# A gated two-layer kernel on one core: 66 instead of 128 weight columns for the low part of g, and another warm-up series

## The reference, cut to what matters

```python
def _attn_ref(x, weight):              # x (4, 4096, 192), weight (8, 7)
    w = softmax(weight)                # over the 7 taps of each head
    x_pad = zeros(6 rows) + x          # along the sequence
    out[b, s, h, g] = sum_k w[h, k] * x_pad[b, s + k, h, g]

def _moe_ref(x, w_in, w_out):          # (16384, 192), (192, 2048), (2048, 192)
    h = x @ w_in
    g = h * np.cos(h)
    return (g @ w_out).astype(np.float32)

def _moe2_ref(x, w_in, w_out):
    h = x @ w_in
    relu6 = np.clip(h + 3.0, 0.0, 6.0)
    g = h * relu6 / 6.0
    return (g @ w_out).astype(np.float32)

def reference(...):
    return _moe2_ref(_moe_ref(_attn_ref(x, weight)))
```

## Time and profile before

| what | value |
|---|---|
| median of 3 runs | 2409.83 us (2409.76 to 2409.97) |
| the profiled execution's own time | 2408.54 us |
| its span | 2406.8 us |
| mean granted clock of TensorE | 0.995 of full |
| busy: TensorE, weight loads | 2367.1 us, 1929.2 us |
| busy: VectorE, ScalarE, GpSimd | 1776.7 us, 1495.7 us, 1313.7 us |
| products, each with its weight load | 10,254 |

### The profile page before, as it was taken

The page is one execution under the profiler, slowest core; times in us unless marked ns, Lnnn a source line. Parts: engine busy times, 40 slices in busy tenths (PEclk is TensorE's granted clock), DMA queues, the critical chain, the costliest instruction groups (busy, mean ns, idle before and its releaser), DMA issues.

```text
span 2406.8 us, 32826 instructions
## 1 busy us (share of the span) xinstructions
PE 2367.1 (98%) x10254; PEld 1929.2 (80%) x10254; DVE 1776.7 (74%) x2253; ACT 1495.7 (62%) x1748; POOL 1313.7 (55%) x543
## 2 busy tenths in 40 slices
PE   5999999999999999999999999999999999999998
PEld 3788888888888888888888888888888888888886
DVE  8777776777767777767777677777677776777753
ACT  4765566665666655666656666566666566665663
POOL 6755555555555555555555555555555555555554
PEclk8999999999999999999999999999999999999999
DMA  4100000000000000000000000000000000000001
GB/s 110 38 1 13 7 7 13 13 13 13 0 13 13 13 13 7 7 13 13 13 13 0 13 13 13 13 6 7 13 13 13 13 0 13 13 13 13 3 4 20
DMA packets 208226, 32.76 MB, mean 14 GB/s; under 512 B 203088, under 2 KB 207184, under 8 KB 208208
## 3 DMA queue, kind: packets, MB, share of 16 engines
q1 hardware_dynamic: 208208, 32.53, 7.7%
HBM read 19.92 MB, written 12.58 MB: 14 GB/s over the span
## 4 chain that ended last, share of the span: by engine, by line
PE 97%; DVE 1%; issue 1%; DMA 1%; SPq 0%; ACT 0%; POOL 0%; DVEq 0%; POOLq 0%; ACTq 0%
PE h_ps L347 10%; PE h_ps L346 10%; PE acc L366 10%; PE acc_tail L368 10%; PE h_ps L349 10%; PE acc L365 10%; PE acc_tail L369 10%; PE h_ps L348 10%; PE h_ps L350 10%; PE acc L367 10%; DMA gate<-in_moe_w_out 1%; DVE pre L520 0%; DVE gate L533 0%; DVE in_ftail L580 0%; DVE in_f L580 0%
## 5 line engine op out<-in xcount | busy, mean ns | idle before, releaser
L690 POOL TENSOR_TENSOR g_lo<-gate,g_hi 128x1024 fp32r<-128x1024 f32 x512 | 1270.2, 2481 | 1070.0 <-ACT g_hi L442 1069.7
L428 ACT ACTIVATE pre<-h_ps,three 128x1024 f32<-128x1024 f32 x256 | 286.7, 1120 | 547.0 <-PE h_ps L350 547.0
L442 ACT ACTIVATE g_hi<-gate 128x1024 fp32r<-128x1024 f32 x512 | 538.8, 1052 | 31.7 <-DVE gate L533 31.2
L520 DVE TENSOR_TENSOR pre<-pre,h_ps 128x1024 f32<-128x1024 int32 x256 | 311.9, 1218 | 257.3 <-ACT pre L426 257.3
L535 DVE SCALAR_TENSOR_TENSOR gate<-pre,h_ps 128x512 f32<-128x512 f32 x512 | 327.3, 678 | 214.5 <-ACT pre L428 213.5
L533 DVE TENSOR_TENSOR gate<-pre,h_ps 128x512 f32<-128x512 f32 x512 | 331.6, 685 | 129.4 <-ACT pre L436 126.0
L346 PE MATMUL h_ps<-in_hi,win_hi 128*128 128x512 f32 x1024 | 406.1, 397 | 18.7 <-DVE gate L533 9.9
L426 ACT ACTIVATE pre<-h_ps 128x1024 int32<-128x1024 f32 x256 | 262.4, 1025 | 232.5 <-PE h_ps L350 232.5
L347 PE MATMUL h_ps<-in_lo,win_hi 128*128 128x512 f32 x1024 | 406.1, 397 | 0.0
L349 PE MATMUL h_ps<-in_tail,wtail_hi 128*128 128x512 f32 x1024 | 403.4, 394 | 0.0
L366 PE MATMUL acc<-g_lo,wout 128*128 128x512 f32 x1024 | 402.6, 393 | 0.0
(11 more groups left out here) (69 smaller groups left out, 2225.8 us busy)
## 6 DMA issues: line engine op xcount, KB each, us to landing
x_in<-in_x SPq DMA_DIRECT2D x128, 64.0 KB, 2.2
out_dram<-o_blk SPq DMA_DIRECT2D x128, 64.0 KB, 1.8
blk_tail<-in_x SPq DMA_DIRECT2D x64, 64.0 KB, 2.2
out_dram<-blk_tail SPq DMA_DIRECT2D x64, 64.0 KB, 1.8
stage<-in_moe_w_out SPq DMA_DIRECT2D x6, 384.0 KB, 3.2
stage<-in_moe_w_in SPq DMA_DIRECT2D x3, 512.0 KB, 3.7
stage<-in_moe_w_in SPq DMA_DIRECT2D x6, 256.0 KB, 4.1
gate<-in_moe_w_out SPq DMA_DIRECT2D x2, 384.0 KB, 12.2
```

The lines of the kernel that those rows point to most:

```text
L442: act.activation(g_hi[:, q % G_BUFS, :], gate[:, q % 2, :], ACT.Copy).then_inc(ghi_ready, 1)
L690: pool.tensor_tensor(g_lo[:, n, :], gate[:, q % 2, :], g_hi[:, n, :].bitcast(F32), ALU.subtract).then_inc(glo_ready, 1)
```

## The change

Two things are changed.

1. In `second_product` the low part of g is multiplied with the 64 columns of the tail's high part and 2 more columns (`NARROW = 66`) instead of all 128. The product of the low part of g with 62 of the 64 columns of the tail's low part is no longer computed. In the last half of a phase the narrow product comes ahead of the wide one, so that the wide one ends the sum on all 128 partitions.
2. `warm_up` waits for the first rounded weights as before, and for the taps' copies (`taps_ready`) instead of nine convolution steps. It issues 62 products instead of ten: whole ones (128 rows, 128 columns), pairs of two that use rows 0 to 63 and rows 64 to 127 into two banks, four with 66 columns and four with 64.

```diff
-WARM_PRODUCTS = 10
-WARM_STEP = 9
+NARROW = 66
...
-                    pe.matmul(acc_tail[pair][:, :], w[:, P:2 * P], hi, start=first, stop=False)
-                    last = pe.matmul(acc_tail[pair][:, :], w[:, P:2 * P], lo, start=False, stop=final)
+                    if not final:
+                        pe.matmul(acc_tail[pair][:, :], w[:, P:2 * P], hi, start=first, stop=False)
+                    last = pe.matmul(acc_tail[pair][0:NARROW, :], w[:, P:P + NARROW], lo, start=False, stop=False)
+                    if final:
+                        last = pe.matmul(acc_tail[pair][:, :], w[:, P:2 * P], hi, start=False, stop=True)
                 last.then_inc(mix_done, 1)
...
                 pe.wait_ge(whi_done, 1)
-                pe.wait_ge(conv_step, WARM_STEP)
-                for _ in range(WARM_PRODUCTS):
-                    pe.matmul(h_ps[:, 1, TOK:W], win_hi[L1][:, 0:P], win_hi[L1][:, 0:TOK], start=True, stop=True)
+                pe.wait_ge(taps_ready, 2)
+                top, low, all_rows = slice(0, DT), slice(DT, P), slice(0, P)
+
+                def product(rows, cols, bank):
+                    pe.matmul(h_ps[0:cols, bank, TOK:W], win_hi[L1][rows, 0:cols], win_hi[L1][rows, 0:TOK],
+                              start=True, stop=True)
+
+                for _ in range(12):
+                    product(all_rows, P, 1)
+                for _ in range(4):
+                    product(top, P, 0)
+                    product(low, P, 1)
+                    for _ in range(3):
+                        product(all_rows, P, 1)
+                for _ in range(6):
+                    product(top, P, 0)
+                    product(low, P, 1)
+                for _ in range(4):
+                    product(all_rows, P, 1)
+                for _ in range(4):
+                    product(all_rows, NARROW, 1)
+                for _ in range(3):
+                    product(all_rows, P, 1)
+                for _ in range(4):
+                    product(all_rows, DT, 1)
+                for _ in range(3):
+                    product(all_rows, P, 1)
```

## The result

The change made the kernel slower: a median of 2423.48 us (2421.99 to 2424.07, six runs) against 2409.90 us (six runs of the kernel before on the same chip). The ratio is 1.0055, 95% interval 1.0042 to 1.0068, so 13.6 us were added. The forecast was no change, 2409.8, within 2392.5 to 2414.0. It was wrong in kind, and the time lies outside the range.

What follows compares the result with a forecast made beforehand. The tensor engine's time from product to product, 230.0 ns, was taken as the bound. Narrow product, order and warm-up summed as 0 + 0 + 0 = 0, giving 2409.8 us, range 2392.5 to 2414.

Steps and rivals of the forecast that it cites:

- The reading of the 17 ns: TensorE's long run: 17 of 230 ns per product are not stream and go with load and product, whatever the width.
- The first rival: In L369 the weight load gates the product, so a narrow load saves 17 ns each: 2393 us, chance 28%.
- its second value: The load-gates-product case by the Trainium skill's page: 14.2 ns saved per narrow product, 14 us in all, 2395 us.
- the second (2401.6): Rival for L369: the 17 ns excess is a share of the load's columns, saving 8 us: 2401.6 us, chance 10%.
- part 1: 66 instead of 128 weight columns in L369, 1024 times: cost 0, bounds 17 us gain and 112 or 223 us loss.
- a broken overlap at 112 us: L369's narrow form not overlapping its neighbours: 0.11 us of a restart once per narrow product, 112 us in all.
- the warm-up's 2414: Upper end of the range, from the new warm-up's bound of +3 us at the start of the kernel.
- The slower rival: At L369 the narrow form breaks the overlap with neighbours, on one side (2522) or both (2633), chance 10%.
- the 0.34 us of a restart: Time from first product to successor when TensorE restarts at 37.03 us, instead of 0.23; expected around L369 if overlap broke.
- Its test: Broken overlap is decided if the gap before or behind L369 grows at all; 5 ns would show.
- Parts 2 and 3: Narrow product before wide in a phase's last half, cost 0; new warm-up, cost 0, bounds -1 and +3 us.
- the expected signs for the start: First real product between 27.04 and 30 us, and VectorE's first subtraction of a fraction still at 34.2 us.

Runs made afterwards that it cites:

- all operands in step: Kernel before with 192 unused bytes ahead of in_f, putting inputs and weights at the same place modulo 256 bytes: 2376.46 us; with the 66-column product too, 2376.58 us.
- distance 64: Inputs left where the kernel before has them, 64 bytes from the weights' place modulo 256 bytes: 2409.95 us for the kernel before.

## Why the prediction was wrong

**The reading of the 17 ns was right.** The load does not gate the product. A load recorded for 0.14 instead of 0.19 gave nothing, neither in the change nor with all operands in step. The first rival (2393, or 2395 by its second value) and the second (2401.6) both fall with this.

**The step that failed is part 1's "cost 0" and its bounds.** I took the excess over the stream's 213 ns as something that goes with a pair of load and product "whatever its width", thus as a constant. It is not: of the 17 ns, 13.3 stay when all operands are in step (226.6 to 226.7), and the other 3.3 are a mean over products that depends on where their operands lie and on the products before them. The narrow slice changed this second part, by 26.7 ns per slot of 20, or 13.3 ns for each narrow product. My bounds had no row for that: 17 ns of gain, and on the other side a broken overlap at 112 us. Between 0 and 112 us I had nothing, so the range ended at the warm-up's 2414.

**The slower rival had the sign and not the mechanism.** No overlap broke: the load of L369 begins with the product before it as ever, and L369 never stood the 0.34 us of a restart from its neighbours. Its test was the useful part of it: any growth "before or behind L369" decides, since nothing covers it. The growth was behind, in the five products that follow the first narrow one of a slot, 1.13 to 1.16; these 25 ns are nearly all of the slot's 26.7.

**The rows could have warned me.** The kernel before had groups of five at 1.13 and at 1.16 in every slot. I checked that the mean was 230.0 over 10,090 products, and took a mean for a pace. A group that is faster than its twins, with the same shapes, says that something else than shape has a part in the time.

**Parts 2 and 3 were right.** The order cost nothing (ratio 1.0000), and so did the warm-up (1.0000). Its series ended at 28.7, inside 26.2 to 34.1. The weight loads of its last part show what the changes of form cost:

```profile
22.62 1.24 PEld L408 LDWEIGHTS h_ps<-win_hi 64*128 64x128 f32 x12 [0.37 <-issue]
24.22 4.01 PEld L408 LDWEIGHTS h_ps<-win_hi 128*128 128x128 f32 x18 [0.36 <-issue]
```

Between the pairs of 64 rows and the whole products around them the loads stood still for 0.37 and 0.36 us, where 0.04 is usual (0.24 to 0.37 at all such changes at full clock). The 18 loads behind that are of 128, 66, 128, 64 and 128 columns, and take 4.01 us, thus 0.23 from one to the next: the changes of width cost nothing. The twelve of 64 rows are six pairs, and a pair passes in some 0.23, as one whole product does. The first real product came at 30.29 rather than by 30, and VectorE's subtraction at 35.99 rather than 34.2, because VectorE's steps were slow; the expected signs for the start were bound to one execution, and it varies by 2 us.

**What stays open.** Distance 0 modulo 256 bytes as the fast place of the inputs is shown by four distances and two places of the same distance. But the pads moved the inputs alone, with all weights at 128 past a multiple of 256. The weights' place counts too: with the moving operand where it was, a full slice shifted by 62 or 32 columns cost 9 and 6 us. Whether it is the distance between the two that counts, or that each begins at 128 past a multiple of 256, no run tells; moving inputs, g and weights together would. What in the memory's read path makes it so was not tried. Nor do I have a rule for partial slices: from the same first column, 127 columns cost 3.3 us, 96 cost 4.7 and 66 cost 13.3, while 66 in one half cost 1.7 or nothing. In the kernels moved by 64 and by 192 bytes the 66 columns were free. In the first of these the first products were out of step as well, so neighbours out of step are not enough to make a narrow slice cost; why it costs with the inputs at distance 64 and not at 128 stays open. Widths other than 66 were tried at distance 64 alone.

## What to carry to other kernels

Where TensorE is the bound, compare groups of equal products with each other before you trust a mean: a pace that differs at equal shape can be time to be had. Look at the addresses of the moving operand and of the weights; here a pad of 192 bytes, putting both at the same place modulo 256 bytes, was worth 1.4%. And making a weight slice narrower gave nothing here beside a stream of 512 columns, at any of three distances, and at one of them it cost 13.3 us.

## What the runs showed of the hardware

- A product of 512 columns in fp32r with its own load of 128 weight columns took between 226.6 ns (both operands at distance 0) and 231.3 ns as a mean over the kernel, at full clock throughout, with only addresses and one slice of the weights changed.
- Slots of 20 products repeated to the nanosecond: 4599 to 4600 ns before, 4626 to 4627 after, in each of some 500 slots of both layers, so that neither the work of the other engines nor the layer shows in it.
- The effect has memory. The five second products right behind the first products took 1.16 us where the next five took 1.13, at the same addresses modulo 256 bytes. With the inputs at distance 0 all twenty took 1.13 per five.
- The pace at half clock showed none of this: 426 ns, the stream alone.
- A load of 66 columns is recorded for 0.14 us against 0.19 for 128, and brought nothing: 9,796 products in 2220 us with either.
- In the warm-up's series, changes between 128, 66 and 64 weight columns left the loads 0.23 us apart; a change between 64 and 128 rows left a gap of 0.24 to 0.37.
- VectorE's steps of 0.74 us took up to 2.9 beside GpSimd's subtractions at the start. Which engine was slowed differed: in the trace before, VectorE kept 0.74 for tile 0 and GpSimd's first subtraction took 6.46 us; in the trace after, GpSimd's took 2.94 and four steps of VectorE 2.85 to 2.87. The start of the steady part lay between 68.3 and 70.5 us.
